# Attention, a mixture of experts and a cosine layer on one core: y moved by feature chunks, the second layer started inside the first's last tile

## The chip, the core and the metric

The kernel runs on one core of a Trainium2 chip. The core has TensorE (PE; its weight loads are listed as PEld), VectorE (DVE), ScalarE (ACT), GpSimd (POOL) and SyncE (SP), which here only issues DMA transfers. Each engine takes its own instructions in order, and they wait for each other through semaphores. The metric is the device time of one launch in microseconds (us), as the median of several runs.

## The reference, cut to what matters

Three stages follow each other. A linear attention with a state (4 batches, 8 heads, 768 steps, 48 features of a head), a mixture of 8 experts whose weights P come out of 8 rounds of normalising rows and columns, and a layer with h·cos(h). In all that follows, "first layer" is the mixture of experts and "second layer" the last one.

```python
# attention, for every t of 768 steps, batch and head:
    y[t] = q[t] @ state
    state = state + beta[t] * outer(k_n[t], v[t] - k_n[t] @ state)
x = y.transpose(0, 2, 1, 3).reshape(3072, 384)      # feature = head * 48 + d
# first layer
P = exp(x @ w_gate - max); 8 rounds: P /= row sums; P /= column sums; P *= N / E
x1 = sum over e of P[:, e] * (relu(x @ w1[e]) @ w2[e])      # 8 experts, 1024 wide
# second layer
h = x1 @ w_in                                        # 2048 wide
out = (h * cos(h)) @ w_out
```

## The kernel before

**Layout.** Tokens are handled in 6 tiles of 512 (`NT`, `TILE`), features in 3 chunks of 128 partitions (`DC`). A product in full float32 precision is made of three passes: each operand is split into a rounded part and the rest (`xhi` and `xlo`, `whi` and `wlo`, `hhi` and `hlo`), and high·high, high·low and low·high are added in PSUM. ScalarE writes the rounded part, and the rest is a subtraction.

**Attention.** It runs over 6 groups (`NG`) of 4 steps of 64 positions, with two batches side by side on the partitions. A group is one token tile. For every two steps (a half group, `hg`), `move_y` (lines 273 to 285) has SP copy the outputs from `yT`, where a partition is a feature of the head and the heads stand side by side, to `acc`, where a partition is one of 384 features. A head has 48 features, and the chunks of 128 cut some heads in two, so a half group takes 20 transfers (10 for each batch). ScalarE waits for them by count (`MOVES`, lines 56, 800, 806 and 853). For five of the six tiles the first half-pass of the first expert is worked off during the attention (the `early_...` functions). What it leaves in `y_stage` is stored to memory (`store_early`) and fetched back later (`reload`). SP's queue is written out at lines 326 to 357. At step 2 of the last group it has `reload(0)` (line 348), which waits until VectorE has made the low part of tile 0 (`x_lo(0)`, line 1350), and behind it stand the transfers of the last half group. The sixth tile's `x_hi(NT - 1)` on ScalarE (lines 851 to 855, called at line 936) waits for these transfers, `x_lo(NT - 1)` on VectorE follows, and with it TensorE begins that tile (lines 664 to 666).

**First layer.** Sixteen passes (8 experts, 2 halves of 512) of 6 tiles run in loops. A tile is 72 matmuls of 512 columns in eight blocks of nine: four of `mm1(j)` (`up`, lines 605 to 607) and four of `mm2(j)` (lines 634 to 636), in the order mm1(0), mm1(1), mm2(0), mm1(2), mm2(1), mm1(3), mm2(2), mm2(3). ScalarE writes `hhi` (line 957), VectorE `hlo` (line 1406). VectorE multiplies the tile's output by the experts' weights (`py`, line 1439), and GpSimd adds it to `acc` (line 1095). GpSimd also splits the next pass's weights (`split_lo`, line 1054).

**Second layer.** Four passes of 6 tiles. A step `st` is one of four 128-wide chunks j of a tile, so 4·6·4 = 96 steps. TensorE's step is nine matmuls `up2(st)` into the bank `h` or `p_h` (by turns) and nine `down2(st - 2)` (lines 703 to 705). Between them lies a chain on two engines: ScalarE writes `kint` (line 1005, the multiple of 2π), VectorE reduces the argument in two instructions (lines 1492 and 1495; I call them r1 and r2), ScalarE takes the absolute value and the sine (lines 1011 and 1013), VectorE multiplies (line 1507, `gg`; I call it g), ScalarE writes `hhi` (line 995), and GpSimd the rest `hlo` (line 1116). `up2(st)` waits for g of step st - 2, because the bank has to be free, and `down2(st)` for `hlo` of step st. The outputs of a tile are taken out of PSUM by VectorE (`take`, lines 1473 to 1482), three a tile, at steps 2 to 4 and 6 to 7 of every eight. In passes 0 to 2, at steps 3 and 6 of every eight, ScalarE and GpSimd also split a chunk of the next pass's weights.

**Where the layers meet.** The second layer's input is split a tile at a time: `x2_hi` on ScalarE (line 946) and `x2_lo` on VectorE (line 1364). Tiles 0 to 3 are split during the last first-layer pass, tiles 4 and 5 in one piece each after the first eight steps of the second layer (lines 1024, 1025 and 1512, 1513). TensorE begins the second layer with `up2` of steps 0 and 1 (lines 715 and 716) after the last `mm2(3)`. At the end SP stores the six tiles of the result, each as one transfer of 768 KB (lines 392 to 394).

## Time and profile before

| | before |
|---|---|
| time, median of 3 runs | 2302.71 us (2301.67 to 2304.5) |
| the profiled execution's own time | 2305.67 us |
| its span in the trace | 2303.9 us |
| TensorE busy | 2220.0 us, 96% of the span |
| VectorE busy | 1014.6 us, 44% |
| ScalarE busy | 742.1 us, 32% |
| GpSimd busy | 687.8 us, 30% |
| DMA, of 16 engines' span | 16.1% |

The page's section on busy time gives each engine's share of the span; the section of 40 slices shows how it is spread. TensorE stands at 9 (90% or more) in nearly all slices from the eighth on, so what can still be won lies in the attention (the first seven slices) and in single gaps of some microseconds, which no average shows. They are found in the order of time: the timeline prints every instruction with its start, its duration and, in brackets, the idle time of its engine before it and what ended it. A matmul is listed with 0.39 us, but consecutive ones start about 0.23 us apart: a gap is read from the starts. The section on the chain that ended last names what released each step. Second-layer rows of GpSimd (line 1116) have 5% of the span there.

### The profile page before, as it was taken

The page shows a single profiled execution, that of the slowest core. Times are in us where ns is not written, and L with a number is a line of the kernel's source. Part 1 is how long each engine was busy: PE and PEld are TensorE (multiplying, and loading weights), DVE is VectorE, ACT ScalarE, POOL GpSimd, SP SyncE. Part 2 cuts the span into 40 slices and gives each one's busy share as a digit, 9 for nine tenths or more (in the row PEclk, how much of TensorE's full clock was granted, in tenths as well). Part 3 has the DMA queues.
Part 4 walks back from the last instruction along what each step waited for, and adds up shares of the span by engine and source line. Part 5 has one row for each costly group of instructions (what it writes and reads, how often), then busy time and mean ns, then how long its engine had stood idle before and what let it go on. Part 6 is the DMA issues. An engine that isn't in the chain of part 4 may idle for free.

```text
span 2303.9 us, 40703 instructions
## 1 busy us (share of the span) xinstructions
PE 2220.0 (96%) x15456; PEld 1845.1 (80%) x15456; DVE 1014.6 (44%) x1641; ACT 742.1 (32%) x1286; POOL 687.8 (30%) x506
## 2 busy tenths in 40 slices
PE   3899998999999999999999999999999999999998
PEld 3788886888888888888888888888888877888887
DVE  8877742643232322322232323232323246767676
ACT  4666542311111111111111111111111126666665
POOL 2100001004432323233332323232323244444433
PEclk9889999999999999999999999999999999999999
DMA  6343333102111011111101111111110100000001
GB/s 160 100 105 98 87 88 118 55 28 55 39 31 29 27 46 32 27 32 27 45 28 32 27 32 27 45 29 30 30 29 27 46 23 14 14 14 14 0 14 69
DMA packets 85221, 102.35 MB, mean 44 GB/s; under 512 B 8384, under 2 KB 70144, under 8 KB 85120
## 3 DMA queue, kind: packets, MB, share of 16 engines
q1 hardware_dynamic: 85120, 100.91, 15.9%
q8 instruction: 75, 1.23, 0.2%
q14 instruction: 26, 0.21, 0.0%
HBM read 87.40 MB, written 8.75 MB: 42 GB/s over the span
## 4 chain that ended last, share of the span: by engine, by line
PE 75%; issue 12%; POOL 6%; DVE 5%; ACT 1%; SPq 1%; DMA 0%; POOLq 0%; DVEq 0%; ACTq 0%
PE p_h L605 5%; PE h L605 5%; PE p_h L606 5%; PE h L606 5%; PE h L607 5%; PE p_h L607 5%; POOL hlo L1116 5%; PE am_y L634 4%; PE am_y L635 4%; PE am_y L636 4%; PE chain_y L634 2%; PE chain_y L635 2%; PE chain_y L636 2%; PE o_y L634 2%; PE o_y L635 2%
## 5 line engine op out<-in xcount | busy, mean ns | idle before, releaser
L1095 POOL TENSOR_TENSOR acc<-acc,py 128x512 f32 (+1 forms) x252 | 325.2, 1321 | 744.4 <-DVE py L1439 744.4
L957 ACT ACTIVATE hhi<-h 128x512 fp32r<-128x512 f32 x182 | 109.0, 599 | 769.5 <-PE h L607 769.5
L1406 DVE SCALAR_TENSOR_TENSOR hlo<-h,hhi 128x512 fp32r<-128x512 f32 x182 | 125.9, 692 | 475.1 <-ACT hhi L957 475.0
L1406 DVE SCALAR_TENSOR_TENSOR hlo<-p_h,hhi 128x512 fp32r<-128x512 f32 x182 | 125.9, 692 | 406.7 <-ACT hhi L957 406.7
L1054 POOL TENSOR_TENSOR wlo<-stage,whi (+1 forms) x117 | 160.4, 1373 | 440.5 <-ACT whi L845 415.6
L605 PE MATMUL h<-xhi,whi 128*128 (+1 forms) x690 | 269.7, 391 | 2.9 <-DVE scr L1507 2.9
L605 PE MATMUL p_h<-xhi,whi 128*128 (+1 forms) x690 | 269.2, 390 | 0.1
L606 PE MATMUL h<-xlo,whi 128*128 (+1 forms) x690 | 269.2, 390 | 0.0
L607 PE MATMUL h<-xhi,wlo 128*128 (+1 forms) x690 | 269.1, 390 | 0.0
L607 PE MATMUL p_h<-xhi,wlo 128*128 (+1 forms) x690 | 268.5, 389 | 0.0
L606 PE MATMUL p_h<-xlo,whi 128*128 (+1 forms) x690 | 268.5, 389 | 0.0
L957 ACT ACTIVATE hhi<-p_h 128x512 fp32r<-128x512 f32 x182 | 109.0, 599 | 435.3 <-PE p_h L607 435.3
L1116 POOL TENSOR_TENSOR hlo<-scr,hhi 128x512 fp32r<-128x512 f32 x96 | 145.6, 1516 | 222.7 <-ACT hhi L995 222.7
L605 PEld LDWEIGHTS h<-xhi,whi 128*128 128x128 f32 x690 | 130.1, 189 | 31.3 <-issue 4.1
L605 PEld LDWEIGHTS p_h<-xhi,whi 128*128 128x128 f32 x690 | 129.5, 188 | 28.5 <-DVE scr L1507 1.8
L607 PEld LDWEIGHTS h<-xhi,wlo 128*128 128x128 f32 x690 | 130.0, 188 | 27.2
L607 PEld LDWEIGHTS p_h<-xhi,wlo 128*128 128x128 f32 x690 | 129.5, 188 | 27.0
L606 PEld LDWEIGHTS h<-xlo,whi 128*128 128x128 f32 x690 | 129.8, 188 | 26.6
L606 PEld LDWEIGHTS p_h<-xlo,whi 128*128 128x128 f32 x690 | 129.6, 188 | 26.6
L634 PE MATMUL am_y<-hhi,whi 128*128 128x512 f32 x368 | 143.2, 389 | 0.0
L635 PE MATMUL am_y<-hlo,whi 128*128 128x512 f32 x368 | 143.2, 389 | 0.0
L636 PE MATMUL am_y<-hhi,wlo 128*128 128x512 f32 x368 | 143.2, 389 | 0.0
(242 smaller groups left out, 4078.1 us busy)
## 6 DMA issues: line engine op xcount, KB each, us to landing
stage<-wcat SPq DMA_DIRECT2D x40, 768.0 KB, 4.4
pb<-p_scratch SPq DMA_DIRECT2D x84, 256.0 KB, 4.6
kq<-kqt SPq DMA_DIRECT2D x48, 192.0 KB, 3.4
kn<-krow SPq DMA_DIRECT2D x6, 768.0 KB, 6.2
kT<-kta SPq DMA_DIRECT2D x24, 192.0 KB, 5.3
v<-vrow SPq DMA_DIRECT2D x24, 192.0 KB, 4.2
kb<-krow SPq DMA_DIRECT2D x24, 192.0 KB, 4.9
out<-acc SPq DMA_DIRECT2D x6, 768.0 KB, 3.8
```

What stands on the lines that cost most here:

```text
L605: pe.matmul(hps[bank][:, 0:TILE], w1(whi, buf, d, j), x_h, start=(d == 0), stop=False)
L606: pe.matmul(hps[bank][:, 0:TILE], w1(whi, buf, d, j), x_l, start=False, stop=False)
L607: mm = pe.matmul(hps[bank][:, 0:TILE], w1(wlo, buf, d, j), x_h, start=False, stop=(d == DC - 1))
L634: pe.matmul(y, w2(whi, half, j, d), hhi[:, j, :], start=(j == 0), stop=False)
L635: pe.matmul(y, w2(whi, half, j, d), hlo[:, j, :], start=False, stop=False)
L636: mm = pe.matmul(y, w2(wlo, half, j, d), hhi[:, j, :], start=False, stop=(j == CH - 1))
L957: act.activation(hhi[:, j, :], hps[j % 2][:, 0:TILE], ACT.Relu).then_inc(s["hhi_done"], 1)
L1054: pool.tensor_tensor(wlo[buf][:, c], stage[:, c], whi[buf][:, c].bitcast(F32), ALU.subtract).then_inc(s["wlo_done"], 1)
L1095: pool.tensor_tensor(y, y, py[:, d, :], ALU.add).then_inc(s["added"], 1)
L1116: pool.tensor_tensor(hlo[:, j, :], gg[:, j % 2, :], hhi[:, j, :].bitcast(F32), ALU.subtract).then_inc(s["h2_split"], 1)
L1406: dve.scalar_tensor_tensor(out=hlo[:, j, :], in0=hps[j % 2][:, 0:TILE], scalar=0.0, in1=hhi[:, j, :].bitcast(F32), op0=ALU.max, op1=ALU.su ...
```

## The change

**y moves by chunks.** The features of x are put in another order: of every head the first 16 go to chunk 0, the next 16 to chunk 1, the last 16 to chunk 2. A chunk is then 16 partitions of `yT` with all 8 heads, and one transfer fills its 128 partitions of `acc`: 6 transfers a half group (`MOVES`), 64 KB each. The rows of `w_gate` and `w1` are put in the same order on the host (`by_chunk`).

**`reload(0)`** stands behind the attention's last `move_y` in SP's queue.

**The second layer begins earlier.** TensorE's `up2` of step 0 goes between mm1(3) and mm2(2) of the last first-layer tile (`final`), and VectorE makes r1, r2 and g of step 0 ahead of that tile's three `py` (`before_y`). To allow it, the last pass's loops are written apart for its last tiles, and `x2_lo(3)` moves into the last tile, behind its third `hlo` (`after_third`).

**`hlo` of the second layer** (`split_h2`) is made by VectorE, one step late, between r2 and the takes or g of the next step. GpSimd keeps only the splits of the weights in the second layer.

**x tiles 4 and 5** are split in chunks (`x2_hi_part`, `x2_lo_part`), one at each of steps 1, 4 and 7 (`X2_AT`) of the first and the second eight steps.

**The last store** is three transfers of one chunk each.

```diff
+X2_AT = (1, 4, 7)
-MOVES = 2 * (HEADS + DC - 1)
+MOVES = 2 * DC
+HP = P // HEADS
...
             sp.wait_ge(a["y_evac"], 2 * hg + 2)
+            col = hg // 2 * 2 * GB + hg % 2 * HB
             for b in range(2):
-                for h in range(HEADS):
-                    f, src = h * HD, b * CT
-                    while f < (h + 1) * HD:
-                        n = min((h + 1) * HD, (f // P + 1) * P) - f
...
+                for c in range(DC):
+                    sp.dma_start(acc[:, c, col + b * GB:col + b * GB + HB],
+                                 yT[b * CT + c * HP:b * CT + (c + 1) * HP, hg % 2, :, :]).then_inc(a[f"y_moved{hg % 2}"], 16)
...
-                if c == 2 and g == NG - 1:
-                    reload(0)
                 if c % 2 == 1:
                     move_y(i // 2)
+        reload(0)
         store_early(EARLY - 1)
...
+        for d in range(DC):
+            sp.wait_ge(s["y2_evac"], (PASSES2 * NT - 1) * DC + d + 1 + 6)
+            sp.dma_start(out[:, d, (NT - 1) * TILE:], x_part(NT - 1, d)).then_inc(s["stored"], 16)
...
             mm1(3)
+            if final:
+
+                pe.wait_ge(s["h_split"], g * CH + 5)
+                pe.wait_ge(s["wlo_done"], PASSES1 * NT + NT // 2)
+                up2(0, 0, 0, 0)
             mm2(2)
             mm2(3)
...
             if q == 0:
-                pe.wait_ge(s["wlo_done"], PASSES1 * NT + NT // 2)
-                up2(0, buf, 0, 0)
                 up2(0, buf, 1, 1)
...
+        def x2_hi_part(t, d):
+            act.wait_ge(s["added"], (PASSES1 * NT - NT + t) * DC + 2 * DC)
+            act.activation(xhi[:, t, d, :], x_part(t, d), ACT.Copy).then_inc(s["x2hi"], 1)
...
-                if st > 0:
+                if st > 0 and not (first and st == 1):
                     hi_of(t0 + (st - 1) // CH, (st - 1) % CH)
...
+                if first and st == 0:
+                    hi_of(0, 0)
+                if x2 is not None and st in X2_AT:
+                    x2_hi_part(NT - 2 + x2, X2_AT.index(st))
...
-        for q in range(PASSES2):
+        for q in range(PASSES2 - 1):
             with pool.Fori(0, NT // 2) as tp:
-                for st in range(2 * CH):
-                    j = st % CH
-                    pool.wait_ge(s["hhi2_done"], (q * NT + tp * 2) * CH + st + 1)
-                    pool.tensor_tensor(hlo[:, j, :], gg[:, j % 2, :], hhi[:, j, :].bitcast(F32),
-                                       ALU.subtract).then_inc(s["h2_split"], 1)
-                    if q < PASSES2 - 1 and st in SPLITS:
-                        split_lo((q + 1) % 2, tp * 2 + SPLITS.index(st), PASSES1 + q + 1)
+                for k in range(2):
+                    split_lo((q + 1) % 2, tp * 2 + k, PASSES1 + q + 1)
...
+        def x2_lo_part(t, d, n):
+            dve.wait_ge(s["x2hi"], NT - 2 + n)
+            ins = dve.tensor_tensor(xlo[:, t, d, :], x_part(t, d), xhi[:, t, d, :].bitcast(F32), ALU.subtract)
+            if d == DC - 1:
+                ins.then_inc(s["x2_done"], 1)
+
+        def split_h2(j, g):
+            dve.wait_ge(s["hhi2_done"], g + 1)
+            dve.tensor_tensor(hlo[:, j, :], gg[:, j % 2, :], hhi[:, j, :].bitcast(F32), ALU.subtract).then_inc(s["h2_split"], 1)
+
+        def steps(q, tp, prev, first=False, x2=None):
...
+                if not (first and st == 0):
+                    reduced(j, g)
+                if st > 0 and not (first and st == 1) or st == 0 and prev:
+
+                    split_h2((st - 1) % CH, g - 1)
                 if prev and 2 <= st < 5:
                     take(*prev, 1, st - 2)
...
+                if not (first and st == 0):
+                    gated(j, g)
+                else:
+                    split_h2(0, 0)
+                if x2 is not None and st in X2_AT:
+                    d = X2_AT.index(st)
+                    x2_lo_part(NT - 2 + x2, d, x2 * DC + d + 1)
+
+
+        tile(N_EXP - 1, 1, 2, 1, WEIGHED, before_y=lambda: (reduced(0, 0), gated(0, 0)), after_third=lambda: x2_lo(3))
```

`reduced` holds r1 and r2, `gated` holds g, with the waits that they had before.

**SP at the end of the attention, before.** The first row stores an early tile, the second is `reload(0)`, the rest is the last half group's moves.

```order
L298 DMA y_scratch<-y_late 128x1536
L304 DMA acc<-y_scratch 128x3x512
L283 DMA acc<-yT 48x128 x2
L283 DMA acc<-yT 32x128
L283 DMA acc<-yT 16x128
L283 DMA acc<-yT 48x128 x2
L283 DMA acc<-yT 16x128
L283 DMA acc<-yT 32x128
```

Twelve more transfers of these shapes follow, and then the store of the fifth tile (line 298) and the next weights. The same place after the change:

```order
L282 DMA acc<-yT 128x1x128 x6
L296 DMA y_scratch<-y_late 128x1536
L282 DMA acc<-yT 128x1x128 x6
L302 DMA acc<-y_scratch 128x3x512
L296 DMA y_scratch<-y_late 128x1536
L287 DMA stage<-wcat 128x1536 x2
```

The reload has moved from ahead of the last moves to behind them, and the moves of a half group have become six rows of 128 partitions.

**VectorE where the layers meet, before.** `py` belongs to the last first-layer tile, `xlo` is x2_lo(3), then come r1, r2 and g of the second layer's steps 0 and 1.

```order
L1439 TENSOR_TENSOR py<-am_y,pb 128x512
L1364 ISA
L1364 REGISTER_ALU
L1364 TENSOR_TENSOR xlo<-acc,xhi 128x1536
L1468 REGISTER_ALU
L1468 COMPARE_AND_BRANCH
L1492 SCALAR_TENSOR_TENSOR scr<-scr,h 128x512
L1495 SCALAR_TENSOR_TENSOR scr<-scr 128x512
L1507 TENSOR_TENSOR scr<-h,scr 128x512
L1492 SCALAR_TENSOR_TENSOR scr<-scr,p_h 128x512
```

After the change, from x2_lo(3) on (line 1377; `hlo` of line 1419 is the first layer's fourth, of line 1526 the second layer's):

```order
L1377 TENSOR_TENSOR xlo<-acc,xhi 128x1536
L1419 SCALAR_TENSOR_TENSOR hlo<-p_h,hhi 128x512
L1506 SCALAR_TENSOR_TENSOR scr<-scr,h 128x512
L1509 SCALAR_TENSOR_TENSOR scr<-scr 128x512
L1516 TENSOR_TENSOR scr<-h,scr 128x512
L1456 TENSOR_TENSOR py<-chain_y,pb 128x512
L1456 TENSOR_TENSOR py<-am_y,pb 128x512 x2
L1526 TENSOR_TENSOR hlo<-scr,hhi 128x512
L1506 SCALAR_TENSOR_TENSOR scr<-scr,p_h 128x512
L1509 SCALAR_TENSOR_TENSOR scr<-scr 128x512
L1516 TENSOR_TENSOR scr<-p_h,scr 128x512
L1520 TENSOR_TENSOR xlo<-acc,xhi 128x512
```

Step 0's r1, r2 and g stand ahead of the three `py`, the second layer's first `hlo` behind them, and the first chunk of tile 4 behind g of step 1.

**VectorE in the second layer, before,** steps 6 and 7 of the first eight, with the takes of a tile and the two whole tiles of x behind them.

```order
L1492 SCALAR_TENSOR_TENSOR scr<-scr,h 128x512
L1495 SCALAR_TENSOR_TENSOR scr<-scr 128x512
L1479 COPY acc<-o_y 128x512
L1507 TENSOR_TENSOR scr<-h,scr 128x512
L1492 SCALAR_TENSOR_TENSOR scr<-scr,p_h 128x512
L1495 SCALAR_TENSOR_TENSOR scr<-scr 128x512
L1479 COPY acc<-state_y 128x512
L1479 COPY acc<-y_y 128x512
L1507 TENSOR_TENSOR scr<-p_h,scr 128x512
L1364 TENSOR_TENSOR xlo<-acc,xhi 128x1536 x2
```

After, step 7 of the same eight and what follows it:

```order
L1506 SCALAR_TENSOR_TENSOR scr<-scr,p_h 128x512
L1509 SCALAR_TENSOR_TENSOR scr<-scr 128x512
L1526 TENSOR_TENSOR hlo<-scr,hhi 128x512
L1497 COPY acc<-state_y 128x512
L1497 COPY acc<-y_y 128x512
L1516 TENSOR_TENSOR scr<-p_h,scr 128x512
L1520 TENSOR_TENSOR xlo<-acc,xhi 128x512
```

Between r2 and g there is now an `hlo`, ahead of the takes, and one chunk of x in the place of two whole tiles.

## Rows read from the trace of the kernel before

**Rows 1.** Windows: stretch, length, busy (x count) by engine, PE clock, DMA.

```profile
core 0: us, PE busy (x) PEld busy (x) DVE busy (x) ACT busy (x) POOL busy (x), PEclk, DMA share, GB/s
400.00:404.00 4.00, 3.92 (x10) 1.48 (x11) 0.02 (x1) 0.00 (x0) 0.00 (x0) 0.52 0.76 310
1000.00:1350.00 350.00, 350.00 (x1546) 289.91 (x1545) 101.90 (x148) 62.43 (x107) 108.05 (x85) 1.00 0.13 34
1899.00:1902.00 3.00, 3.00 (x8) 2.34 (x7) 1.47 (x3) 1.51 (x3) 1.71 (x1) 0.50 0.03 5
1904.40:1938.80 34.40, 31.51 (x136) 24.98 (x135) 22.88 (x27) 22.21 (x34) 15.72 (x10) 1.00 0.00 1
1938.80:2289.80 351.00, 350.19 (x1529) 285.73 (x1530) 248.78 (x319) 220.29 (x357) 155.13 (x101) 1.00 0.05 18
```

**Rows 2.** Timeline of SP, end of the attention: start, length of the issues, count.

```profile
382.10 0.64 SPq L304 DMA_DIRECT2D acc<-y_scratch  x1
382.83 12.61 SPq L283 DMA_DIRECT2D acc<-yT  x20
```

**Rows 3.** Timeline of ACT and PE at the same place, bracket: idle before.

```profile
376.69 0.60 ACT L801 ACTIVATE yT<-y_y 128x512 f32<-128x512 f32 x1 [0.44 <-PE y_y L562]
393.35 0.60 ACT L839 ACTIVATE y_late<-o_y 128x512 f32<-128x512 f32 x1 [3.10 <-PE o_y L486]
396.75 1.48 ACT L862 ACTIVATE xhi<-acc 128x1536 fp32r<-128x1536 f32 x1 [2.80 <-DMA acc<-yT]
400.08 0.59 PE L466 MATMUL o_y<-xhi,wgr 128*8 128x512 f32 x1 [6.77 <-DVE xlo L1273]
```

**Rows 4.** Timeline of PE and POOL where the layers meet.

```profile
1895.73 0.39 PE L607 MATMUL p_h<-xhi,wlo 128*128 128x512 f32 x1
1898.63 0.61 PE L605 MATMUL h<-xhi,whi 128*128 x1 [2.52 <-DVE scr L1507]
1891.74 5.73 POOL L1095 TENSOR_TENSOR acc<-acc,py 128x512 f32 x3 [9.30 <-DVE py L1439]
```

**Rows 5.** Timeline of ACT, DVE and PE at the whole tiles of x.

```profile
1927.45 2.85 ACT L946 ACTIVATE xhi<-acc 128x1536 fp32r<-128x1536 f32 x2
1928.96 3.43 DVE L1364 TENSOR_TENSOR xlo<-acc,xhi 128x1536 fp32r<-128x1536 f32 x2 [0.69 <-ACT xhi L946]
1933.56 0.50 PE L703 MATMUL chain_y<-hhi,whi 128*128 128x512 f32 x1 [2.35 <-POOL hlo L1116]
```

**Rows 6.** Timeline of ACT, DVE and POOL, three steps of the third pass.

```profile
2133.35 0.72 ACT L1013 ACTIVATE scr<-scr,halfpi 128x512 f32<-128x512 f32 x1
2136.82 0.72 ACT L1013 ACTIVATE scr<-scr,halfpi 128x512 f32<-128x512 f32 x1
2137.58 0.69 DVE L1507 TENSOR_TENSOR scr<-p_h,scr 128x512 f32<-128x512 f32 x1 [1.46 <-ACT scr L1013]
2139.67 1.67 DVE L1495 SCALAR_TENSOR_TENSOR scr<-scr 128x512 f32<-128x512 int32 x1
2139.51 1.28 POOL L1116 TENSOR_TENSOR hlo<-scr,hhi 128x512 fp32r<-128x512 f32 x1 [2.23 <-ACT hhi L995]
```

**Rows 7.** Lines 1495 and 1278: count, ns min/median/max, first and last start.

```profile
L1495 DVE SCALAR_TENSOR_TENSOR scr<-scr x96: 691/694/1819, 1895.5 to 2291.6; 128x512 f32<-128x512 int32 x96
L1278 DVE TENSOR_TENSOR wlo<-stage,whi x3: 682/683/692, 35.7 to 36.9; 128x512 fp32r<-128x512 f32 x3
```

**Rows 8.** Waits of the whole span: us in total, times, longest.

```profile
DVE scr L1507 <- ACT scr L1013: 98.5, 96, 1.5
```

**Rows 9.** Timeline of PE and POOL, the last two steps.

```profile
2293.50 0.50 PE L703 MATMUL chain_y<-hhi,whi 128*128 128x512 f32 x1 [1.22 <-POOL hlo L1116]
2296.53 0.50 PE L703 MATMUL chain_y<-hhi,whi 128*128 128x512 f32 x1 [0.69 <-POOL hlo L1116]
```

**Rows 10.** DMA issues: count, KB each, median us from issue to landing.

```profile
out<-acc SPq DMA_DIRECT2D x6, 768.0 KB, 3.8
acc<-yT SPq DMA_DIRECT2D x144, 24.0 KB, 1.8
```

More of the change, by code:

```diff
@@ L608, in up, with up2, tile @@
             return mm
-        def tile(e, half, tp, k, mode):
+        def up2(tile, buf, j, g):
+            pe.wait_ge(s["g_done"], g + 1)
+            if j == 0:
+                pe.wait_ge(s["x2_done"], tile + 1)
+            up(tile, buf, j, j % 2).then_inc(s["mm1b"], 1)
+        def tile(e, half, tp, k, mode, final=False):
             g = (e * 2 + half) * NT + tp * 2 + k
@@ L689, in _ @@
                         tile(e, half, tp, k, WEIGHED)
-        def up2(tile, buf, j, g):
-            pe.wait_ge(s["g_done"], g + 1)
-            if j == 0:
-                pe.wait_ge(s["x2_done"], tile + 1)
-            up(tile, buf, j, j % 2).then_inc(s["mm1b"], 1)
+        with pe.Fori(0, NT // 2) as tp:
+            for k in range(2):
+                tile(N_EXP - 1, 0, tp, k, WEIGHED)
+        with pe.Fori(0, NT // 2 - 1) as tp:
+            for k in range(2):
+                tile(N_EXP - 1, 1, tp, k, WEIGHED)
+        for k in range(2):
+            tile(N_EXP - 1, 1, NT // 2 - 1, k, WEIGHED, final=k == 1)
         def down2(tile_in_pair, buf, j, g, tile_no):
@@ L995, in hi_of, with steps @@
             act.activation(hhi[:, j, :], gg[:, j % 2, :], ACT.Copy).then_inc(s["hhi2_done"], 1)
-        def steps(q, tp, first):
+        def steps(q, tp, first, x2=None):
             t0 = q * NT + tp * 2
@@ L1005, in steps @@
                 act.activation(kint[:, j % 2, :], hps[j % 2][:, 0:TILE], ACT.Copy, scale=INV_2PI).then_inc(s["k_done"], 1)
-                if st > 0:
+                if st > 0 and not (first and st == 1):
                     hi_of(t0 + (st - 1) // CH, (st - 1) % CH)
-                elif not first:
+                elif st == 0 and not first:
                     hi_of(t0 - 1, CH - 1)
@@ L1022, in _ @@
             if q == 0:
-                steps(0, 0, True)
-                for t in range(NT - 2, NT):
-                    x2_hi(t)
-            with act.Fori(1 if q == 0 else 0, NT // 2) as tp:
+                steps(0, 0, True, x2=0)
+                steps(0, 1, False, x2=1)
+            with act.Fori(2 if q == 0 else 0, NT // 2) as tp:
                 steps(q, tp, False)
@@ L1388, in columns, with tile @@
                               ALU.mult).then_inc(s["sunk"], 1)
-        def tile(e, half, tp, k, mode):
+        def tile(e, half, tp, k, mode, after_third=None, before_y=None):
             g = (e * 2 + half) * NT + tp * 2 + k
@@ L1467, in _ @@
             tile(N_EXP - 1, 1, 0, k, WEIGHED)
-        with dve.Fori(1, NT // 2) as tp:
-            for k in range(2):
-                tile(N_EXP - 1, 1, tp, k, WEIGHED)
-                x2_lo(tp * 2 + k - 2)
+        for k in range(2):
+            tile(N_EXP - 1, 1, 1, k, WEIGHED)
+            x2_lo(k)
+        tile(N_EXP - 1, 1, 2, 0, WEIGHED)
+        x2_lo(2)
         def take(q, tile, bank, t):
@@ L1503, in steps @@
                     take(q, tp * 2, 0, 2)
[L1504 to L1507 removed]
+                if not (first and st == 0):
[6 more added lines that the diff above has]
+        tile(N_EXP - 1, 1, 2, 1, WEIGHED, before_y=lambda: (reduced(0, 0), gated(0, 0)), after_third=lambda: x2_lo(3))
         for q in range(PASSES2):
[L1510 removed]
+            steps(q, 0, (q - 1, NT - 1) if q else None, first=q == 0, x2=None if q else 0)
             if q == 0:
[L1512 to L1514 removed]
+                steps(0, 1, (0, 1), x2=1)
+            with dve.Fori(2 if q == 0 else 1, NT // 2) as tp:
                 steps(q, tp, (q, tp * 2 - 1))
+        split_h2(CH - 1, PASSES2 * NT * CH - 1)
         for t in range(DC):
@@ L1548, with by_chunk @@
     half = D_FF // FP
-    up = moe_w1.reshape(N_EXP, DC, P, half, FP).transpose(0, 3, 2, 1, 4).reshape(PASSES1, P, DC * FP)
+    def by_chunk(a):
+        split = a.reshape(*a.shape[:-2], HEADS, DC, HP, a.shape[-1])
+        return np.moveaxis(split, -4, -2).reshape(a.shape)
+    up = by_chunk(moe_w1).reshape(N_EXP, DC, P, half, FP).transpose(0, 3, 2, 1, 4).reshape(PASSES1, P, DC * FP)
     down = moe_w2.reshape(PASSES1, CH, P, D_MODEL).transpose(0, 2, 1, 3).reshape(PASSES1, P, CH * D_MODEL)
```

47 lines of the change are left out of this document (22 added, 25 removed).

## The prediction

> **What bounds the kernel now.** I read the windows first: from the first layer on TensorE is busy all the time and its clock is at the higher of its two levels (granted 1.00, 2.4 GHz). A stretch of the first layer, 350 us with 1546 matmuls [rows 1], gives the pace to measure every other stretch by: 350/1546 = 0.2264 us a matmul, so nine take 2.04 us and a step of the second layer, with eighteen, takes 4.08 us. A change can win only where TensorE falls behind this pace. Then I read the timeline for the places where it does. There are five, and the change touches each.
>
> 1. End of the attention. TensorE stands 6.77 us and waits for the sixth tile's `xlo`; its `xhi` waited 2.80 us for the moves of y [rows 3]. The moves' issue begins only at 382.83, behind the reload of 382.10, and takes 12.61 us [rows 2], although y was ready at 376.69 + 0.60 = 377.3 [rows 3].
> 2. Where the layers meet. From 1895.73 to 1898.63 TensorE waits for g of step 0; one pace taken off, 2.67 us [rows 4]. From 1899 to 1902 the granted clock is 0.50, that is 1.2 GHz [rows 1], so half of 3.00 us is lost: 1.5. Together 4.2.
> 3. The next 34.4 us, to 1938.8: 136 matmuls would take 30.8, so 3.6 are lost [rows 1]. The largest piece is a wait of 2.35 us, behind 2.85 us on ScalarE and 3.43 us on VectorE for two whole tiles of x [rows 5].
> 4. The rest of the second layer, 351.0 us. The weight loads, one for each matmul, count 1530 (one matmul's record is missing), which at the pace take 346.4: 4.6 lost [rows 1].
> 5. The end: TensorE waits 1.22 and 0.69 us for GpSimd's `hlo` [rows 9], and the last 768 KB need 3.8 us from issue to landing [rows 10].
>
> **Why place 4 loses time.** Sine to sine, two steps follow each other in 2136.82 - 2133.35 = 3.47 us when the chain runs free [rows 6]; below 4.08 TensorE would never wait. But r2 takes 0.69 us in one step and 1.67 in another, in which GpSimd's `hlo` of 1.28 us started 0.16 us before it [rows 6]; over the layer the median is 0.694 and the longest 1.819 [rows 7]. Such a step takes 3.47 + 0.98 = 4.45 us. The mixture is near 4.08, and TensorE is held by a few tenths now and then.
>
> The Trainium skill, "SBUF — State Buffer", section "Who interferes with whom", says that a VectorE instruction with two inputs in SBUF contends with a GpSimd instruction that reads SBUF, and that the second to issue is blocked until the first is through. The trace agrees (1.67 against 0.69). By that rule the new `hlo` on VectorE is itself open to this, against the splits of the weights, and a collision could cost the whole 1.28 rather than the 0.98 of the row; four collisions in place 3 would then cost 5.1 in place of 3.9.
>
> **The change, place by place.**
>
> *Place 1.* With the reload behind them, the moves are issued from 377.3. The issue cost of one is 12.61/20 = 0.63 us [rows 2]; six take 3.8, to 381.1. A transfer of 64 KB is not in the trace. It lands between 1.8 us (24 KB) and 3.8 us (768 KB) after its issue [rows 10]; even the longer gives 384.9. ScalarE is busy with the fifth tile's outputs until 393.35 + 0.60 = 393.95 [rows 3], so 9 us of cover lie above the moves, and `xhi` starts at 393.95 in place of 396.75: 2.8 us gained. What comes last then is ScalarE's output, and TensorE still stands 6.77 - 2.8 = 4.0 us. After its idle of 6.77 us the clock was at 0.52 from 400 to 404 [rows 1], which cost 0.48 · 4.00 = 1.9. After 4.0 us I expect the same, since 2.52 us were enough at place 2. In the attention itself the freed SP time gains nothing: no engine's wait between 60 and 390 us ends on a transfer, and the moved reload still waits for `x_lo(0)`, as before.
>
> *Place 2.* TensorE issues the same blocks up to the end of up2(1), so that end stays at 1895.96. The chain of step 0 now runs under mm2(2), mm2(3) and up2(1), three blocks of 2.04, so the 4.2 us go. What is late next is g of step 1: up2(2) and down2(0) fill 4.08 us, and up2(3) could start at 1900.04. The last matmul of up2(1) ends at 1895.73 + 0.39 = 1896.12 [rows 4]. From `kint` to the end of g it is a free loop plus g's tail less the sine that stands before `kint`: 3.47 + (2137.58 + 0.69 - 2136.82) - 0.72 = 4.20 [rows 6]. So g is there at 1900.3 at the earliest: 0.3 us of new wait. VectorE has three `py` and the `hlo` of step 0 ahead of r1, and GpSimd's three adds (5.73 us in all [rows 4]) fall on this `hlo` and on r2, each by up to 0.98: at most 2.3. I take the middle, 1.3, and a gain of 2.9 (1.9 to 3.9).
>
> *Place 3.* The two whole tiles go, and a chunk of x comes at six steps: 3.43/6 = 0.57 us on VectorE (at most the 0.68 of such a subtraction alone [rows 7]), beside 2.85/6 = 0.48 on ScalarE [rows 5]. Over sixteen steps the chain takes 16 · 3.47 = 55.5, + 6 · 0.68 for x, + 4 · 0.48 for the weights' splits on ScalarE, + 2 · 0.6 where two takes stand behind the `hlo` (3 · 0.68 against an idle of 1.46 [rows 6]) = 62.7, and up to 4 · 0.98 more for collisions: 66.6. TensorE needs 65.3. So the chain is up to 1.3 late, besides the lateness at the start; I take 0.7, and a gain of 2.9 (1.7 to 3.6).
>
> *Place 4.* GpSimd's `hlo` goes, and r2 is back at 0.69 but for 18 splits of weights. VectorE's `hlo` is a subtraction of the same shape as line 1278, 0.68 us [rows 7], and stands where VectorE waits for the sine: 1.46 us without a take [rows 6], 98.5/96 = 1.03 on the mean [rows 8]. With one take, 1.37 still fits; with two, 0.6 sticks out once in eight steps. Eight steps then take 8 · 3.47 + 0.6 + 2 · 0.48 + 2 · 0.98 = 31.3, against 32.6 on TensorE. Nothing is late, and of the 4.6 us I take 4.3, since the loop's own registers keep something (3.0 to 4.6).
>
> *Place 5.* The `hlo` is 0.6 us shorter, twice, but the last g stands behind a split and two takes: 0.3 gained (0 to 1.2). Of the last store only 256 KB follow the last take; on the line between 24 KB in 1.8 and 768 KB in 3.8 us that is 2.4, so 1.4 gained (0.5 to 2.0). Together 1.7.
>
> **Sum.** 2.8 + 2.9 + 2.9 + 4.3 + 1.7 = 14.6 us. The profiled execution, with 2305.67 us (a span of 2303.9 and 1.8 around it), would come to 2291.1; it lies 3 us above the median of 2302.71, from which I count: 2288.1. With all terms at their good ends the gain is 18.1 (2284.6), at their bad ends 9.9 (2292.8).
>
> **The rivals.**
>
> - *The clock stays up at place 1.* An idle of 4.0 us is shorter than 6.77, and one of 2.35 us [rows 5] was followed by a stretch at 1.00 [rows 1]. Against it: the 2.52 us of place 2 were followed by 0.50. It would give 1.9 more: 2286.2. Chance 0.13.
> - *A cold start of the second layer.* The new wait at up2(3) comes to 2.3 us, near the 2.52 after which the clock fell: 1.0 + 1.5 lost, 2290.6. Chance 0.12.
> - *The moves come late.* If a transfer out of 16 partitions were so slow that the six took over 9 us longer than reckoned, place 1 would gain nothing: 2290.9. No row has such a shape; that 24 KB land in 1.8 us speaks against it. Chance 0.04. The Trainium skill, "SBUF — State Buffer", section "Door 1: The DMA port swizzle", says that bandwidth goes by the ports that the partitions reach, and has 104 GB/s for 16 partitions; estimated from that, 64 KB take 0.6 us and six 3.8, still inside the cover. No run here shows it yet.
> - *The change doesn't do what it says at place 4:* r2 stretches for another reason than GpSimd's `hlo`, and 4.3 stay lost, perhaps 2.9 of place 3 too: 2292.4 to 2295.3. The coincidence of the two rows speaks against it. Chance 0.06, half of it with so little gain that it can't be told from none.
> - *VectorE becomes the bound (slower).* If `hlo` doesn't fit under the sine, because it waits for `hhi` on ScalarE, the 0.68 and the six takes of eight steps (0.51 a step) lengthen the loop to 3.47 + 1.19 = 4.66: 0.58 over TensorE's 4.08, times 96 steps, 56 us, 2344. It turns slower than before once a step exceeds 4.08 + 14.6/96 = 4.23, that is with 0.76 us uncovered. Against it: `hhi` is written while r1 and r2 run, and the mean idle of 1.03 is longer than 0.68. Chance 0.05.
>
> **How the numbers follow.** The forecast has 0.60 and gives 2288.1. The range 2284.5 to 2293.0 takes in its bounds, the first three rivals and the better half of the fourth. A measurement of this kernel can tell about 0.2%, 4.6 us, from no change. Faster by more than that: all but half of the fourth rival and the fifth, 0.92; within it 0.03; slower 0.05.
>
> **What would show it.** In the profile after, `xhi` of the sixth tile should start at about 394 with ScalarE, not a transfer, ahead of it; up2(2) should follow up2(1) without a gap and up2(3) wait about 1.3 us; r2 should be 0.69 nearly everywhere; TensorE's matmuls between the layers' meeting and the end should keep 0.2264 us; and the last landing should come some 2.4 us after the last issue. I am wrong if TensorE waits in the second layer step by step for line 1516 or 1526, or if the moves land after 394.

## The result, and the profile after

The changed kernel takes 2287.59 us (median of 4 runs, 2285.48 to 2290.11) against 2303.61 for the kernel before (2301.67 to 2306.24): a ratio of 0.9933, 95% interval 0.9919 to 0.9946. The forecast was 2288.1, in a range of 2284.5 to 2293.0, with 0.92 on faster. The profiled execution of after takes 2286.53 us, with a span of 2284.7.

The page of after: busy time by engine, and the chain that ended last by engine.

```profile
PE 2211.2 (97%) x15456; PEld 1842.6 (81%) x15456; DVE 1034.9 (45%) x1741; ACT 739.6 (32%) x1290; POOL 533.4 (23%) x410
...
PE 82%; DVE 1%; ACT 0%; issue 0%; DVEq 0%
```

TensorE was the bound and is so still more: busy for 97% of the span, where it was 96%. The chain, which this page follows back to 392 us only, hardly leaves it. Place by place, as the prediction numbers them.

*Place 1*, timeline of SP, ACT and PE after the last copy of y (start, length, line, bracket: idle before and who ended it), to be held against [rows 2, 3]:

```profile
373.79 0.60 ACT L812 ACTIVATE yT<-y_y 128x512 f32<-128x512 f32 x1 [0.44 <-PE y_y L562]
374.46 3.79 SPq L282 DMA_DIRECT2D acc<-yT  x6
390.45 0.60 ACT L850 ACTIVATE y_late<-o_y 128x512 f32<-128x512 f32 x1 [3.10 <-PE o_y L486]
390.94 1.47 ACT L873 ACTIVATE xhi<-acc 128x1536 fp32r<-128x1536 f32 x1
394.26 0.59 PE L466 MATMUL o_y<-xhi,wgr 128*8 128x512 f32 x1 [3.85 <-DVE xlo L1286]
```

Six moves are issued in 3.79 us, and `xhi` has no bracket: what stands ahead of it is ScalarE's own row, and no transfer. From the last copy of y to the `xhi` it is 17.15 us, where it was 20.06; TensorE's idle is 3.85 in place of 6.77.

*Places 1, 3 and 4*, windows of after: the slow matmuls behind that idle, and the second layer from its second step to its last two (columns as in [rows 1]).

```profile
394.26:397.66 3.40, 3.40 (x9) 1.07 (x10) 0.00 (x0) 0.00 (x0) 0.00 (x0) 0.52 0.96 376
...
1897.53:2274.80 377.27, 377.27 (x1664) 312.52 (x1665) 289.39 (x443) 241.23 (x395) 23.28 (x18) 1.00 0.05 17
```

The clock still falls to 1.2 GHz behind the idle (0.52). In the second layer 1665 weight loads at the pace of 0.2264 us take 376.9 of the 377.3 us: nothing is left of the waits of places 3 and 4.

*Place 2*, timeline of PE, POOL and DVE where the layers meet, to be held against [rows 4]:

```profile
1889.26 4.70 POOL L1113 TENSOR_TENSOR acc<-acc,py 128x512 f32 x3 [12.70 <-DVE py L1456]
1890.13 0.97 DVE L1526 TENSOR_TENSOR hlo<-scr,hhi 128x512 fp32r<-128x512 f32 x1
1891.73 1.07 DVE L1509 SCALAR_TENSOR_TENSOR scr<-scr 128x512 f32<-128x512 int32 x1
1895.00 0.50 PE L605 MATMUL p_h<-xhi,whi 128*128 x1 [0.68 <-DVE scr L1516]
1897.53 0.50 PE L716 MATMUL o_y<-hhi,whi 128*128 128x512 f32 x1 [0.17 <-DVE hlo L1526]
```

The wait of 2.52 us and the slow matmuls behind it are gone. Two short ones are new: at up2(3) for g of step 1 (start to start 0.83 over the pace, and 0.11 more to the matmul after it: 0.94) and at the next second-half step for `hlo` (0.44). The granted clock stays at 1.00 there, as this window shows:

```profile
1894.00:1898.00 4.00, 3.15 (x13) 2.04 (x12) 3.18 (x5) 2.81 (x6) 0.00 (x0) 1.00 0.00 0
```

*Why*: r2 (line 1509, once line 1495) and `hlo` (line 1526) over the second layer, count and ns min/median/max, to be held against [rows 7].

```profile
L1509 DVE SCALAR_TENSOR_TENSOR scr<-scr x96: 691/692/1066, 1885.6 to 2274.6; 128x512 f32<-128x512 int32 x96
...
L1526 DVE TENSOR_TENSOR hlo<-scr,hhi x96: 681/685/973, 1890.1 to 2278.4; 128x512 fp32r<-128x512 f32 x96
```

The longest r2 was 1819 ns before. Both longest values are those beside GpSimd's adds in the fence of place 2.

*Place 5*, PE's last two waits, SP's last issues, and the issues' landing (count, KB each, median us), to be held against [rows 9, 10]:

```profile
2275.91 0.50 PE L716 MATMUL chain_y<-hhi,whi 128*128 128x512 f32 x1 [0.70 <-DVE hlo L1526]
2279.10 0.50 PE L716 MATMUL chain_y<-hhi,whi 128*128 128x512 f32 x1 [0.84 <-DVE hlo L1526]
...
2280.82 1.73 SPq L394 DMA_DIRECT2D out<-acc  x3
...
out<-acc SPq DMA_DIRECT2D x3, 256.0 KB, 2.1
```

### The profile page after: what moved, and what is told of

Its sections match the earlier page's. It is cut to its first block, busy times and chain, and to the rows that moved or that the text cites. A ratio compares the mean times of both kernels' runs of the same rounds, so it can differ in the third digit from the quotient of the medians.

```text
span 2284.7 us, 40279 instructions
## 1 busy us (share of the span) xinstructions
PE 2211.2 (97%) x15456; PEld 1842.6 (81%) x15456; DVE 1034.9 (45%) x1741; ACT 739.6 (32%) x1290; POOL 533.4 (23%) x410
## 3 DMA queue, kind: packets, MB, share of 16 engines
q1 hardware_dynamic: 82464, 100.89, 16.3%
## 4 chain that ended last, share of the span: by engine, by line
PE 82%; DVE 1%; ACT 0%; issue 0%; DVEq 0%
PE h L605 7%; PE h L606 7%; PE h L607 7%; PE p_h L605 7%; PE p_h L607 7%; PE p_h L606 7%; PE am_y L640 4%; PE am_y L642 4%; PE am_y L641 4%; PE chain_y L640 2%; PE chain_y L641 2%; PE chain_y L642 2%; PE o_y L640 2%; PE state_y L640 2%; PE y_y L641 2%; PE state_y L642 2%
## 5 line engine op out<-in xcount | busy, mean ns | idle before, releaser
L1072 POOL TENSOR_TENSOR wlo<-stage,whi (+1 forms) x117 | 152.0, 1302 | 699.1 <-ACT whi L856 674.1
L1026 ACT ACTIVATE scr<-scr 128x512 f32<-128x512 f32 x96 | 60.8, 633 | 94.5 <-DVE scr L1509 94.5
```

The lines of the kernel that those rows point to most:

```text
L1026: act.activation(rr[:, j % 2, :], rr[:, j % 2, :], ACT.Abs).then_inc(s["abs_done"], 1)
L1072: pool.tensor_tensor(wlo[buf][:, c], stage[:, c], whi[buf][:, c].bitcast(F32), ALU.subtract).then_inc(s["wlo_done"], 1)
```

## Five stages, to be read in every run

Runs of one kernel differ by several us, as much as the parts that are to be told apart. So I cut each trace at four events that all these kernels have: the last copy of y on ScalarE (A ends), TensorE's first matmul on x of the sixth tile (B), the first second-half matmul of the second layer (C), the start of the last matmul (D); E is the rest of the span. In us:

| kernel | A | B | C | D | E | B to E |
|---|---|---|---|---|---|---|
| before | 376.69 | 23.39 | 1502.30 | 396.09 | 5.43 | 1927.2 |
| e0_before, the same again | 374.28 | 23.35 | 1502.35 | 396.04 | 5.48 | 1927.2 |
| after | 373.79 | 20.47 | 1497.86 | 388.94 | 3.64 | 1910.9 |
| e1_reload | 371.50 | 20.47 | 1497.62 | 389.00 | 3.61 | 1910.7 |
| e2_twenty | 368.37 | 20.47 | 1497.64 | 388.97 | 3.55 | 1910.6 |
| e3_both | 374.05 | 23.36 | 1498.08 | 388.98 | 3.63 | 1914.1 |
| e4_pool | 372.18 | 20.46 | 1500.67 | 397.48 | 3.61 | 1922.2 |
| e5_whole | 372.30 | 20.47 | 1497.83 | 390.96 | 3.54 | 1912.8 |
| e6_late | 374.67 | 20.47 | 1501.89 | 387.53 | 3.64 | 1913.5 |
| e7_one | 371.44 | 20.46 | 1497.86 | 389.00 | 5.54 | 1912.9 |
| e8_dummy | 377.10 | 20.48 | 1497.57 | 389.54 | 3.61 | 1911.2 |
| e9_early | 372.46 | 17.40 | 1496.18 | 388.95 | 3.61 | 1906.1 |
| e10_best | 376.62 | 17.43 | 1496.26 | 388.22 | 4.07 | 1906.0 |
| e11_hlo | 369.61 | 23.36 | 1502.50 | 389.96 | 5.47 | 1921.3 |

Stages that a kernel leaves as they were agree within 0.1 us (B, D, E; the span behind E is known to 0.1) or 0.5 (C); A alone scatters, over 8.7 us. From B to E the change brings 1927.2 - 1910.9 = 16.3 us.

## Experiments: what brings the attention's end forward

**The kernel before once more** (no edit).

> The kernel before, once more, for a second profile of it. Theory of the clock: the last copy of y, at 376.69 us in the first profile, moves by up to 3 us with the granted clock of this execution between 90 and 150 us (0.66 in the first profile), and so do the times of its rounds, 2301.7 to 2306.2. Rival (the changed kernel's moves make the attention shorter): the last copy of y stands within 0.5 us of 376.69 again. The other waits are the same: 4.2 us where the layers meet, 3.6 at x of tiles 4 and 5, 4.6 through the second layer. Ratio 1.000.

Measured: 2304.26 us, ratio 1.0001 (0.9988 to 1.0013); the last copy of y 2.4 us earlier than in the first profile, B to E the same 1927.2. Nothing in the kernel changed, so the attention's end moves by itself, and the 2.9 us by which after's attention ended earlier can't be counted as a gain of the change. The next three, and e11 below, say the same: with twenty moves A is 368.4 to 376.7 in five profiles (mean 372.6), with six 371.4 to 377.1 in nine (373.6). What differs most plainly between before and e11_hlo, whose attention is the same code, is the clock. Windows of 110 to 130 us, first of before, then of e11_hlo:

```profile
110.00:130.00 20.00, 20.00 (x482) 19.60 (x480) 11.97 (x30) 10.58 (x23) 0.00 (x0) 0.57 0.24 63
```

```profile
110.00:130.00 20.00, 18.91 (x638) 18.19 (x634) 16.46 (x42) 14.15 (x33) 0.00 (x0) 1.00 0.25 67
```

With a granted clock of 0.57 TensorE comes through 482 matmuls there, with 1.00 through 638. The copies of y of e11_hlo run level with those of before up to 85 us, are 2.1 us ahead at 112 and 6.9 at 135, and 7.1 at the end.

The clock between 90 and 150 us alone, by which I had expected the end to go, doesn't rank the profiles: it is 0.80 in e8_dummy, whose last copy is the latest (377.1), and 0.66 in before. In e8_dummy the copies are 4.3 us ahead of before at 151 us and 0.4 behind at 209. Between lies a stretch in which its clock is down again (window of e8_dummy; before and e11_hlo have 1.00 there, with 673 and 682 matmuls):

```profile
150.00:180.00 30.00, 28.08 (x580) 23.46 (x578) 20.77 (x54) 13.91 (x20) 2.99 (x1) 0.89 0.24 70
```

In these three profiles the scatter so goes with where the clock falls in the attention. Why it falls where it does, no run here tells.

**The read-back ahead of the moves again**, six moves kept.

```
+                if c == 2 and g == NG - 1:
+                    reload(0)
                 if c % 2 == 1:
                     move_y(i // 2)
-        reload(0)
```

> The changed kernel with the read-back of early tile 0 put again ahead of the last six moves of y. In the changed kernel the hi part of x of tile 5 starts 17.15 us after the last copy of y ends up on ScalarE's list (390.94 against 373.79), with ScalarE's own row ahead of it; in the kernel before it was 20.06 us (396.75 against 376.69). Theory (the cover suffices for one of the two cures alone): the six moves are issued some 5.5 us later, from about 380, take 3.8 and land 2.7 later, near 386.5, and the hi part still starts 17.2 us after the last copy; time 2287.6, as the changed kernel. Rival (the read-back ahead of the moves was what cost): 20.0 us and 2290.4. Of the end of the attention, 2.9 us earlier in the changed kernel's profile: if the six moves did it, the last copy is again near 373.8; if the granted clock of that execution did it, it lies anywhere between 373 and 378, and goes with the granted clock between 90 and 150 us.

Measured: 2285.69 us; B is 20.47 as in after, and `xhi` starts 17.15 us after the last copy of y. **Twenty moves again**, the read-back kept behind them: the old `move_y`, the old `MOVES`, and weights and gate packed without `by_chunk`.

> The changed kernel with the old order of the features and its twenty moves of y for half a group; the read-back of tile 0 stays behind the moves. Theory (cover): the twenty moves take 12.61 us of SP's list from the last copy of y, end near 387 if that copy is near 374, and land by 390, just ahead of the 391 at which ScalarE comes to the hi part: it starts 17.2 to 18 us after the last copy; time 2287.6 to 2288.4. Rival (the number of moves was what cost): 20.0 us, 2290.4. End of the attention: if the six moves made it earlier, the last copy is near 376.7 here; if the clock did, it goes with the granted clock between 90 and 150 us (0.66 in the kernel before, 0.74 in the changed one).

Measured: 2287.85 us; B is again 20.47. The moves are issued here for 12.83 us, and `xhi` still has no bracket (timeline of SP and ACT):

```profile
369.04 12.83 SPq L285 DMA_DIRECT2D acc<-yT  x20
...
385.52 1.47 ACT L877 ACTIVATE xhi<-acc 128x1536 fp32r<-128x1536 f32 x1
```

**Both undone.**

> The changed kernel with both undone: twenty moves of y, and the read-back of tile 0 ahead of the last twenty. Theory: the hi part of x of tile 5 again waits for the moves and starts 20.0 us after the last copy of y; 2.8 us slower than the changed kernel, 2290.4. Rival (the moves are hidden here, and the 2.8 us of the prediction came with the earlier end of the attention): 17.2 us and 2287.6. End of the attention as in the run with twenty moves: 376.7 if the moves set it, with the granted clock if that does.

Measured: 2289.95 us; the wait for the moves is back, and B is 2.9 longer (timeline of ACT and PE):

```profile
394.08 1.48 ACT L878 ACTIVATE xhi<-acc 128x1536 fp32r<-128x1536 f32 x1 [2.79 <-DMA acc<-yT]
...
397.41 0.60 PE L471 MATMUL o_y<-xhi,wgr 128*8 128x512 f32 x1 [6.75 <-DVE xlo L1291]
```

So place 1 is worth 2.9 us, and either cure alone brings all of it: the new order of the features, and the read-back moved by a few lines. With both, the last move lands at about 380 us, 11 us before `xhi` starts, and nothing asks for that much cover.

## Experiments: the second layer's parts undone one by one

**`hlo` on GpSimd again** (its loop of the kernel before; VectorE's three calls of `split_h2` taken out).

> The changed kernel with the remainders of the second layer (hlo) on GpSimd again, the rest unchanged. Theory: the shorter step of VectorE is what frees the second layer: with GpSimd's subtraction of some 1.1 us in place of 0.69 and VectorE's second reduction at 1.67 beside it, the loop from one sine to the next is longer than TensorE's 4.08 us wherever two takes stand in it, and the 4.6 us of waits of the kernel before (about 0.2 at every eighth step) come back, with up to 1 us more at the end of the program: 2292 to 2293. Rival (the waits went because the second layer starts earlier and the lists are displaced by one step): 2287.6, and no waits between 1900 and 2270 us.

Measured: 2296.97 us, and 11.3 more from B to E, twice what I expected. The edit makes a new wait where the layers meet. Timeline of POOL and PE there, and r2's line:

```profile
1887.73 4.21 POOL L1113 TENSOR_TENSOR acc<-acc,py 128x512 f32 x3 [12.70 <-DVE py L1461]
1891.90 1.27 POOL L1134 TENSOR_TENSOR hlo<-scr,hhi 128x512 fp32r<-128x512 f32 x1
1893.31 0.49 PE L716 MATMUL o_y<-hhi,whi 128*128 128x512 f32 x1 [2.56 <-POOL hlo L1134]
...
L1514 DVE SCALAR_TENSOR_TENSOR scr<-scr x96: 691/694/1798, 1884.0 to 2283.9; 128x512 f32<-128x512 int32 x96
```

The first `hlo` now stands on GpSimd's list behind the last tile's three adds; TensorE waits 2.56 us and then has a slow stretch. Windows of e4_pool: that stretch, the next 68 us, and the rest.

```profile
1893.30:1898.00 4.70, 4.69 (x14) 3.69 (x15) 3.02 (x4) 1.81 (x3) 1.28 (x1) 0.64 0.00 0
```

```profile
1898.00:1966.00 68.00, 66.49 (x282) 51.76 (x281) 47.87 (x60) 41.64 (x71) 28.35 (x19) 1.00 0.04 12
1966.00:2284.00 318.00, 317.42 (x1390) 259.29 (x1389) 225.12 (x291) 199.74 (x323) 140.51 (x92) 1.00 0.05 18
```

By the weight loads (281 and 1389 at the pace) 4.4 us are lost in the one and 3.5 in the other, and 1.7 in the slow stretch by the clock; with the chunks of x in place, the early steps lose their time again. r2 is back at up to 1.80 us. So the waits did go because `hlo` left GpSimd, and the chunks need that too; the early start and GpSimd's `hlo` don't go together. Whether it is r2 that matters, or the length of `hlo` itself (1.27 us and more on GpSimd, 0.68 on VectorE), this run doesn't tell apart, as it undoes both.

**`hlo` on VectorE in the kernel before**, that part alone.

```
+                if st > 0 or prev:
+                    split_h2((st - 1) % CH, g - 1)
```

> The kernel before with one part of the change alone: the remainders of the second layer (hlo) on VectorE, one step late; GpSimd keeps the weights' lo halves. Read by the time from the last copy of y to the end of the span, which was 1927.2 us in both profiles of the kernel before and 1910.9 in that of the changed kernel (the last copy itself moved between 368.4 and 377.1 us from profile to profile). Theory (the parts add up): the 4.6 us of waits of the steady second layer go; the wait of 3.6 us at x of tiles 4 and 5 falls to the 2.0 that the changed kernel lost when the whole tiles were put back into it, 1.6 less; 0.3 at the end: 6.5 in all, 1920.7. Rival 1 (putting hlo back cost the changed kernel 11.3, so hlo is worth 11.3 in either kernel): 1915.9. Rival 2 (hlo on VectorE pays only together with the chunks of x and the early first step, and alone VectorE's longer list is in the way): 1924 to 1928. By the theory the time is some 6.5 below that of the kernel before in the same rounds, 2294 to 2298.

Measured: 2296.17 us, ratio 0.9972 (0.9959 to 0.9985); 5.9 less from B to E (6.1 less in D, 0.2 more in C): near the 6.5 of the theory, far from 11.3. What the part leaves in the layer (timeline of PE, windows):

```profile
1891.84 0.79 PE L605 MATMUL h<-xhi,whi 128*128 x1 [2.52 <-DVE scr L1508]
1926.38 0.50 PE L703 MATMUL chain_y<-hhi,whi 128*128 128x512 f32 x1 [2.17 <-DVE hlo L1481]
```

```profile
1930.00:2279.00 349.00, 349.00 (x1542) 288.97 (x1541) 266.20 (x407) 220.53 (x359) 20.69 (x16) 1.00 0.05 19
```

The steady part keeps the pace (1541 loads take 348.9 of 349.0); the whole tiles still cost one wait of 2.17.

**Whole tiles of x again** in the changed kernel: `x2_hi` and `x2_lo` of tiles 4 and 5 between the first eight steps and the next, no chunks.

> The changed kernel with x of tiles 4 and 5 split whole between the first eight steps and the next, as in the kernel before, the rest unchanged (hlo on VectorE). Theory: two whole tiles on ScalarE (2 x 1.5) and on VectorE (2 x 1.7) stand between two steps again and TensorE waits some 2.9 to 3.6 us there: 2290.5 to 2291.2. Rival (with hlo on VectorE the lists have spare time enough to take it): under 1 us, 2287.6 to 2288.6.

Measured: 2290.83 us; D is 2.0 longer, less than the 2.9 to 3.6 I expected, in one wait of the same 2.17 us that e11_hlo has. The clock doesn't fall behind it (timeline of PE, window):

```profile
1922.46 0.50 PE L716 MATMUL chain_y<-hhi,whi 128*128 128x512 f32 x1 [2.17 <-DVE hlo L1528]
```

```profile
1922.46:1925.46 3.00, 3.00 (x13) 2.46 (x14) 2.17 (x4) 2.01 (x5) 0.00 (x0) 1.00 0.00 0
```

Of the 3.6 us of place 3 `hlo` on VectorE thus brings some 1.6 and the chunks 2.0.

**The first step behind the last tile again**, in the changed kernel.

```
-            if final: ... up2(0, 0, 0, 0)
             mm2(2)
             mm2(3)
+            if final: ... up2(0, 0, 0, 0)
...
-        tile(..., before_y=lambda: (reduced(0, 0), gated(0, 0)), ...)
+        tile(..., ...)
+        reduced(0, 0)
+        gated(0, 0)
```

> The changed kernel with the second layer's first step behind the first layer's last tile again: its matmuls after the last second-half matmuls of that tile, its reduction and gate behind that tile's results on VectorE; x of tile 4 and 5 in chunks and hlo on VectorE stay. Theory: the first reduction's chain is bare again and TensorE waits some 3 us where the layers meet, with a stretch at the lower clock or without: 2.0 to 3.6 slower than the changed kernel, 2289.6 to 2291.2. Rival (the wait moves to another step and costs as much in the changed kernel): 2287.6 to 2288.5.

Measured: 2290.86 us; C is 4.0 longer and D 1.4 shorter, as the two new short waits go: 2.6 net. Timeline of PE and the window behind the wait:

```profile
1893.28 0.67 PE L605 MATMUL h<-xhi,whi 128*128 x1 [2.33 <-DVE scr L1516]
```

```profile
1893.30:1896.70 3.40, 3.40 (x8) 2.67 (x9) 1.98 (x3) 1.77 (x4) 0.00 (x0) 0.52 0.00 0
```

**One store at the end**: the kernel before's loop over all six tiles.

> The changed kernel with the last tile stored in one transfer instead of three. Theory: the last issue is no later, but the one transfer lands 3.8 us after its issue (as in the kernel before) in place of 2.1: 1.4 to 1.7 us slower at the end of the span, 2289.0 to 2289.3. Rival (the issue of three costs what the smaller ones save): equal, 2287.6.

Measured: 2287.15 us, which tells nothing; E is 5.54 in place of 3.64, so the three small transfers bring 1.9 us, a little over the 1.4 to 1.7 expected.

## Experiments: room on VectorE, and a faster version

**A second subtraction behind each `hlo`**, from the second pass on.

```
                     split_h2((st - 1) % CH, g - 1)
+                    if q:
+                        dve.tensor_tensor(py[:, 0, :], gg[:, (st - 1) % 2, :], hhi[:, (st - 1) % CH, :].bitcast(F32), ALU.subtract)
```

> The changed kernel with a second subtraction of the same size as hlo on VectorE behind every hlo from the second pass of the second layer on (71 or 72 of them; its result is read by nobody). Theory: VectorE's work in a step is on average 3.3 us of 4.08 (four operations of 0.69 and 6 takes of 0.69 in eight steps); with 0.69 more it is 3.96 and still under the step, but in the steps with two takes 4.8 us stand in one loop and TensorE waits up to 0.5 us in each pass over two tiles, nine times: 2287.6 to 2292. Rival (VectorE is the bound already, the changed kernel only just fits): each of the 72 adds most of its 0.69, 40 us and more: 2325 and over.

Measured: 2288.41 us. Window of the steady part and PE's last wait:

```profile
2000.00:2270.00 270.00, 270.00 (x1193) 223.58 (x1192) 242.23 (x382) 171.12 (x276) 15.54 (x12) 1.00 0.05 16
```

```profile
2282.75 0.50 PE L716 MATMUL chain_y<-hhi,whi 128*128 128x512 f32 x1 [1.45 <-DVE hlo L1526]
```

VectorE is busy 242 of 270 us (90%) and TensorE keeps the pace (1192 loads take 269.9); only the last wait is 0.6 longer. Even the nine steps with two takes lose nothing. From the second pass on, the changed kernel has room for one more operation of 0.69 us a step.

**`xhi` of the sixth tile two results earlier** on ScalarE's list.

```
         for d in range(DC):
             early_out(t, d)
-        x_hi(NT - 1)
+            if d == 0:
+                x_hi(NT - 1)
```

> The changed kernel with one more step: on ScalarE the hi part of x of tile 5 stands after the first of the three results of early tile 4 instead of after the third. The moves have landed by about 381 us and the row is idle for over 1.6 us between these results, so it costs ScalarE's list nothing, and VectorE's lo is long done when TensorE ends the early tile. Theory: TensorE's wait of 3.85 us for that lo falls to the 0.6 to 0.9 us of the last result's own evacuation, and with so short a stop the granted clock doesn't fall, which gives the 1.9 us at 1.2 GHz back: 3 to 5 us, 2282.6 to 2284.6. Rival (the next thing is late: the logits of tile 5 wait for ScalarE's copies of o_y, or tile 5's hidden rows for theirs): under 1.5 us, 2286.1 to 2287.6.

Measured: 2282.26 us (2280.03 to 2285.88), ratio to before 0.9919 (0.9905 to 0.9933); B is 3.1 and C 1.7 shorter. Timeline of ACT and PE, and the first matmuls' window:

```profile
382.21 1.48 ACT L873 ACTIVATE xhi<-acc 128x1536 fp32r<-128x1536 f32 x1
385.42 0.60 ACT L850 ACTIVATE y_late<-o_y 128x512 f32<-128x512 f32 x1 [1.72 <-PE o_y L486]
...
389.86 0.39 PE L466 MATMUL o_y<-xhi,wgr 128*8 128x512 f32 x1 [0.78 <-ACT y_late L850]
```

```profile
389.86:393.26 3.40, 3.40 (x15) 1.99 (x16) 0.00 (x0) 0.59 (x1) 0.00 (x0) 1.00 0.84 244
```

ScalarE still waits 1.72 us for the next result, so the place in its list was free; TensorE's idle is 0.78, and the clock stays at 2.4 GHz. From B to E this kernel is 4.8 us under the changed kernel and 21.1 under the kernel before. By the times alone it isn't told apart from the changed kernel for sure, as the two intervals overlap.

**The last two second-half steps with `hhi`'s matmuls first**, on top of that: `down2` waits for `hhi2_done`, runs the matmuls by `hhi` (of all three results, in the last step of two), then waits for `h2_split`.

> The kernel of the run before with one more step: in the last two second-half steps of the program the matmuls that read hhi stand ahead of those that read hlo, as none of the next step's work is left to cover hlo. Theory: the two waits for hlo at the end, 0.85 and 1.0 us, fall to 0.1 to 0.3 each; 1.0 to 1.6 less than the run before, too little for the rounds to tell and to be read from the trace: 2281.2 to 2283.2. Rival (VectorE's takes at the end come later by as much, as the three results of the last tile end closer together): 0 to 0.5 us less.

Measured: 2284.57 us; D is 0.7 shorter, E 0.5 longer. The rival held: TensorE's last wait is now for `hhi`, and the last takes end as late.

```profile
2276.59 0.50 PE L714 MATMUL chain_y<-hhi,whi 128*128 128x512 f32 x1 [1.12 <-ACT hhi L1032]
```

## Why the prediction was right, point by point

- *Place 1, 2.8 us: measured 2.9* (B; e3_both). Issue from the copy of y, 3.8 us for six, ScalarE last, an idle of 4.0 (3.85) and a clock of 0.52 behind it: each as written. The six moves, of which no row had the shape, landed 2.4 us after their issue (median), by about 380 us, so the rival that they come late is out. So is the rival that the clock stays up; e9_early shows what that would have brought, 1.7 in C against the 1.9 reckoned. The attention itself shows no gain, as said; its 2.9 us in the profile of after lie within the scatter.
- *Place 2, 2.9 us: measured 3.1* (C -4.4, and 1.4 of new waits in D; e6_late 2.6). The wait came at up2(3) as named, with 0.94 where I took 1.3, and a second of 0.44 that I had not listed. Mis-sized was the collision with GpSimd's adds: up to 0.98 each for `hlo` and r2, measured 0.97 - 0.68 = 0.29 and 1.07 - 0.69 = 0.38; each met only the last part of an add. The cold start didn't happen: the longest new wait is 0.68.
- *Place 3, 2.9 us: measured 3.6*, the whole loss. I charged up to four collisions of r2 with the weights' splits. All 18 splits start 0.3 to 0.5 us ahead of r1, which has one input in PSUM and keeps its 0.69 beside them. When r2 starts they are through but for less than 0.1 us, save the first, whose last 0.27 us fall on an r2 (0.82). A split waits for ScalarE's half of it, which stands right behind a sine, and r1 for the `kint` behind that, so the splits fall on the same place of the step every time. The first of them, timeline of POOL and DVE:

```profile
1902.49 1.29 POOL L1072 TENSOR_TENSOR wlo<-stage,whi  x1 [8.53 <-ACT whi L856]
...
1902.79 0.69 DVE L1506 SCALAR_TENSOR_TENSOR scr<-scr,h 128x512 f32<-128x512 int32 x1 [0.31 <-ACT scr L1020]
1903.51 0.82 DVE L1509 SCALAR_TENSOR_TENSOR scr<-scr 128x512 f32<-128x512 int32 x1
```

  The Trainium skill, "SBUF — State Buffer", section "Who interferes with whom", has the second of two such instructions blocked until the first is through. The trace agrees: an r2 or `hlo` that starts beside a running GpSimd instruction ends 0.55 us after that one's end, in [rows 6] (2141.34 against 2140.79) as in the fence above (1904.33 against 1903.78), so a collision costs what is left of the first, less 0.14. The 5.1 us that I worked out by the rule did not come because the splits all but miss r2, and not because the rule fails.
- *Place 4, 4.3 us: measured 4.6*, all of it within 0.3; what I left to the loop's registers rested on no row. `hlo` fits beside the sine, and the step with two takes needs no time of TensorE. That the loss came from `hlo` on GpSimd is shown (e4_pool, e11_hlo). That it came by r2 alone, as I reckoned, is not: of TensorE's eleven waits in this stretch before, six of some 0.3 us end on GpSimd's `hlo` and five shorter ones on g. One of the six, timeline of DVE, POOL and PE of before:

```profile
2131.96 0.69 DVE L1495 SCALAR_TENSOR_TENSOR scr<-scr 128x512 f32<-128x512 int32 x1
2132.16 1.64 POOL L1116 TENSOR_TENSOR hlo<-scr,hhi 128x512 fp32r<-128x512 f32 x1 [1.82 <-ACT hhi L995]
2133.86 0.50 PE L703 MATMUL chain_y<-hhi,whi 128*128 128x512 f32 x1
```

  Here r2 came first and kept its 0.69, and `hlo` (1.28 in [rows 6]) was held to 1.64: it ends at 2133.80, and the matmul starts at 2133.86, 0.29 late. The steps before had two r2 of 1.78 and 1.68. Over the 96 steps r2 was held 42 times and `hlo` 54 times, and I had counted only the first. How the 4.6 us divide between them stays open. The rivals "doesn't do what it says" and "VectorE becomes the bound" are out, the second by a wide margin (e8_dummy).
- *Place 5, 1.7 us: measured 2.2.* The store is worth 1.8 to 1.9 (E), as it landed 2.1 us after its issue where I took 2.4; the two waits for `hlo` fell from 1.91 to 1.54, though the last one grew from 0.69 to 0.84 behind the two takes.

The sum is 2.9 + 3.1 + 3.6 + 4.6 + 2.2 = 16.4 (16.3 by the stages) against 14.6: every term was a little low, in places 2 and 3 because I took the middle of bounds whose bad ends were collisions that don't occur. That the median lies within 0.5 us of the forecast is luck in part: the gain was 1.4 us larger than forecast by the times (16.0), and the median of before, from which I had counted, has come out 0.9 higher with one more run (2303.61 for 2302.71). A alone moves a run by several us.

## What to carry to other kernels

Read the bound engine's pace from a quiet stretch, count its instructions in every other stretch, and price each wait from there; sizes read like that add up within 0.1 us here (16.4 against 16.3), and those priced beforehand were 1.7 short in all. Before reordering data to make a transfer cheaper, look whether moving one unrelated transfer out of its way already hides it, and which engine's list comes last behind it: a row moved two places up that list (e9_early) was worth more than the reordering. And try a part alone as well as taken out: `hlo` was worth 5.9 us put into the old kernel and 11.3 taken out of the new one, because the early start and the chunks of x had come to need it.
